# Attention, experts and a dense layer on one core: moving operands prepared over other steps, and a new order of the first slots

## What is computed

```python
# attention, batch 2, 8 heads, 768 tokens, 64 features per head
scores_l = scale * q @ k^T            # kept where |i - j| < 16, else -1e9
scores_s = scale * q @ max(k, blocks of 32)^T + log(32)
a = softmax(concat(scores_l, scores_s))
x = (a @ concat(v, mean(v, blocks of 32)))            # -> x: 1536 tokens x 512
# four experts, hidden 1024 each
x = sum_e p[:, e] * (relu(x @ w1[e]) @ w2[e])         # p: normalised domain_probs
# dense layer, hidden 2048
h = x @ w_in
out = (h * sigmoid(1.702 * h)) @ w_out
```

## Time and profile before

| | us |
|---|---|
| median of 3 runs | 871.56 (871.52 to 872.74) |
| the profiled execution | 872.22 |
| its span in the profile | 870.4 |
| PE busy in the span | 829.6 (95%) |
| POOL busy | 561.2 (64%) |
| DVE busy | 532.2 (61%) |
| ACT busy | 400.1 (46%) |

### The profile page before, as it was taken

The page is one execution under the profiler, slowest core; times in us unless marked ns, Lnnn a source line. Parts: engine busy times, 40 slices in busy tenths (PEclk is TensorE's granted clock), DMA queues, the critical chain, the costliest instruction groups (busy, mean ns, idle before and its releaser), DMA issues.

```text
span 870.4 us, 13892 instructions
## 1 busy us (share of the span) xinstructions
PE 829.6 (95%) x5032; PEld 809.2 (93%) x5032; DVE 532.2 (61%) x1193; ACT 400.1 (46%) x861; POOL 561.2 (64%) x420
## 2 busy tenths in 40 slices
PE   5975999999999999999999999997999998999998
PEld 3765999999999999899999999997999998999998
DVE  4755556666566566566566665664565654566665
ACT  2654544445444444433344333444455545455441
POOL 3567756566556689757556575799466699556550
PEclk9977999999999999999999999999999999999999
DMA  9971242152111211212213121121112121312102
GB/s 270 290 172 55 91 131 83 49 185 78 49 50 55 110 49 57 107 49 99 66 49 116 49 93 53 49 97 49 49 52 94 49 81 66 121 50 97 49 2 73
DMA packets 26420, 74.72 MB, mean 86 GB/s; under 512 B 14704, under 2 KB 15856, under 8 KB 20208
## 3 DMA queue, kind: packets, MB, share of 16 engines
q1 hardware_dynamic: 26352, 73.84, 26.3%
HBM read 70.66 MB, written 3.17 MB: 85 GB/s over the span
## 4 chain that ended last, share of the span: by engine, by line
PE 81%; POOL 9%; issue 4%; ACT 2%; DVE 2%; DMA 1%; SPq 0%; ACTq 0%; DVEq 0%; POOLq 0%
PE bank L1041 26%; PE bank L1043 26%; PE bank L1042 26%; POOL xb_other_lo L527 2%; PE bank L996 1%; POOL t_late L548 1%; DMA k_win<-k_w 1%; POOL wd_lo L513 1%; PE bank L1033 1%; POOL wu_lo L507 1%; PE bank L1007 1%; POOL prob L470 1%; POOL xb_first_lo L527 1%; POOL stage L492 1%; POOL w_sum L490 1%
## 5 line engine op out<-in xcount | busy, mean ns | idle before, releaser
L860 DVE TENSOR_TENSOR xa<-bank,xa 128x384 f32<-128x384 f32 x352 | 195.8, 557 | 219.2 <-PE bank L1043 214.9
L1041 PE MATMUL bank<-h_hi,wd_hi 128*128 128x384 f32 x768 | 258.1, 336 | 0.1
L1043 PE MATMUL bank<-h_lo,wd_hi 128*128 128x384 f32 x768 | 257.7, 335 | 0.0
L1042 PE MATMUL bank<-h_hi,wd_lo 128*128 128x384 f32 x768 | 257.6, 335 | 0.0
L513 POOL TENSOR_TENSOR wd_lo<-stage,wd_hi 128x1024 fp32r<-128x1024 f32 x48 | 115.0, 2396 | 184.9 <-ACT wd_hi L656 184.9
L695 ACT ACTIVATE h_hi<-bank 128x384 fp32r<-128x384 f32 x192 | 94.4, 492 | 224.5 <-DVE bank L891 176.6
L1041 PEld LDWEIGHTS bank<-h_hi,wd_hi 128*128 128x128 f32 x768 | 145.0, 189 | 1.0 <-issue 1.0
L1043 PEld LDWEIGHTS bank<-h_lo,wd_hi 128*128 128x128 f32 x768 | 145.0, 189 | 0.0
L1042 PEld LDWEIGHTS bank<-h_hi,wd_lo 128*128 128x128 f32 x768 | 145.0, 189 | 0.0
L1041 PE MATMUL bank<-xb_other_hi,wu_hi 128*128 128x384 f32 x336 | 112.4, 334 | 5.7 <-ACT snap L679 5.7
L501 POOL TENSOR_TENSOR wu_lo<-stage,wu_hi 128x1024 fp32r<-128x1024 f32 x48 | 114.9, 2395 | 0.0
(11 more groups left out here) (79 smaller groups left out, 1318.4 us busy)
## 6 DMA issues: line engine op xcount, KB each, us to landing
stage<-weights SPq DMA_DIRECT2D x48, 1024.0 KB, 4.9
k_win<-k_w SPq DMA_DIRECT2D x8, 720.0 KB, 8.9
v_win<-v_w SPq DMA_DIRECT2D x8, 576.0 KB, 8.7
q_bd<-q_t SPq DMA_DIRECT2D x16, 192.0 KB, 9.0
p_bc<-p_rows SPq DMA_DIRECT2D x8, 384.0 KB, 4.8
v_cols<-v_t SPq DMA_DIRECT2D x6, 384.0 KB, 6.5
out<-xa SPq DMA_DIRECT2D x4, 384.0 KB, 7.6
out<-xa SPq DMA_DIRECT2D x8, 192.0 KB, 1.9
```

The costliest lines, as they stand in the source:

```text
L860: nc.vector.tensor_tensor(at, y_bank(g, t), at, ALU.add).then_inc(y_taken, 1)
L1041: nc.tensor.matmul(dst, w_h, a_h, start=first, stop=False, skip_group_check=True)
L1042: nc.tensor.matmul(dst, w_l, a_h, start=False, stop=False, skip_group_check=True)
L1043: return nc.tensor.matmul(dst, w_h, a_l, start=False, stop=last, skip_group_check=True)
```

## The change

It does five things. (1) The parts of phases 2 and 3 are made over six steps ahead of the phase (26 to 31, 34 to 39), and nothing of them in the phase's first step; phase 1 keeps its four steps 13 to 16, with its instructions in other places of POOL's and ACT's queues, none of them behind `low_down`. (2) In phase 0 the token halves swap roles (`tokens`), the first step runs its products in the order P1, P5, P6, P2, P7, P4, P3, P1 and P5 of it stand in slots 15 and 16, and the weights of steps 0 and 1 are made earlier in the queues; DVE makes all low parts and sums of phase 0. (3) ACT copies the turned weights of groups 3 to 11, DVE those of 0 to 2. (4) `key_maxima` of a unit stands one slot later, that of unit 1 two slots later; `probs` is loaded ahead of the first values, and `normalize_weights` stands in slot 1. (5) At the end of step 13 ACT runs a sigmoid of one column, before which the sigmoid table is loaded.

```diff
-MADE_0 = (0, 2, 1, 3, 4, 6, 5)
-MADE = (0, 1, 2, 6, 3, 4, 5)
+MADE = (0, 2, 3, 1, 4, 5, 6)
+ORDER_0 = ("P1", "P5", "P6", "P2", "P7", "P4", "P3")
+AHEAD = (None, 3, 6, 6)
...
+        def keys_due(slot):
+            return [1] if slot == GROUPS else [u for u in unit_starting(slot, -1) if u > 1]
...
         def on_act(k):
-            return k >= B_GROUPS or k % 4 == 3
+            return k >= GROUPS
...
+        def tokens(c):
+            return slice(HALF * (1 - c), HALF * (2 - c))
...
         def preparing(g):
-            return next(((ph + 1, g - LAST[ph] + 2) for ph in range(3) if -1 <= LAST[ph] - g < 3), (None, None))
+            return next(((ph, g - FIRST[ph] + AHEAD[ph]) for ph in range(1, 4)
+                         if FIRST[ph] - AHEAD[ph] <= g < FIRST[ph] + (ph == 1)), (None, None))
...
             sp.dma_start(cst[:], consts).then_inc(const_in, 16)
+            sp.dma_start(dp[:], probs.rearrange("(p t) e -> p t e", p=P)).then_inc(dp_in, 16)
...
-            sp.dma_start(dp[:], probs.rearrange("(p t) e -> p t e", p=P)).then_inc(dp_in, 16)
...
 # POOL, slots
-                if slot == 3 + L_X:
+                if slot == 10:
                     sum_weights(0)
-                if slot == 4 + L_X:
+                if slot == 11:
                     low_raw(0)
-                if slot == 5 + L_X:
-                    low_moved(0, 0)
-                if slot == 6 + L_X:
-                    sum_first()
-                if slot == 7 + L_X:
+                if slot == 13:
                     low_sums(0)
-                if slot == 8 + L_X:
-                    low_moved(0, 2)
-            spread_key_maxima(KT)
-            low_down(0)
+                if slot == 14:
+                    low_down(0)
 # POOL, steps
                 ph, part = preparing(g)
-                if part == 3:
-                    low_moved(ph, 4)
+                soon = ph == 1
+                if soon and part == 3:
                     low_moved(ph, 5)
+                    low_moved(ph, 6)
                 if g + 1 < STEPS:
                     sum_weights(g + 1)
+                    if g == 0:
+                        spread_key_maxima(KT)
                     low_raw(g + 1)
...
                 if part == 0:
                     sum_moved(ph, 1)
                 if part == 1:
-                    sum_moved(ph, 2)
+                    low_moved(ph, 2 if soon else 0)
                 if part == 2:
-                    low_moved(ph, 3)
-                    sum_moved(ph, 3)
+                    sum_moved(ph, 4 if soon else 3)
+                if part == 3 and not soon:
+                    sum_moved(ph, 4)
+                if part == 4:
+                    low_moved(ph, 4)
+                if part == 5:
+                    low_moved(ph, 6)
                 if g + 1 < STEPS:
                     low_sums(g + 1)
...
                 if part == 0:
-                    low_moved(ph, 0)
+                    sum_moved(ph, 2)
+                    if soon:
+                        low_moved(ph, 0)
                 if part == 1:
-                    low_moved(ph, 2)
+                    if soon:
+                        sum_moved(ph, 3)
+                        low_moved(ph, 3)
+                    else:
+                        low_moved(ph, 2)
                 if part == 2:
-                    sum_moved(ph, 4)
+                    if soon:
+                        low_moved(ph, 1)
+                        low_moved(ph, 4)
+                    else:
+                        low_moved(ph, 3)
+                if part == 3 and not soon:
+                    low_moved(ph, 1)
+                if part == 4:
+                    low_moved(ph, 5)
                 if g + 1 < STEPS:
                     low_down(g + 1)
-                if part == 0:
-                    low_moved(ph, 1)
-                if part == 1:
-                    low_moved(ph, 6)
...
 # ACT, slots and step 0
-                if slot == 4 + L_X:
+                if slot == 11:
                     high_raw(0)
+                if slot == 12:
+                    high_sums(0)
                     high_moved(0, 0)
-                if slot == 6 + L_X:
-                    high_sums(0)
-                if slot == 7 + L_X:
+                if slot == 14:
+                    high_down(0, 0)
+                    high_down(0, 1)
                     high_moved(0, 2)
-                if slot == 10 + L_X:
-                    high_moved(0, 1)
-            for i in MADE_0[3:]:
+                if slot == 16:
+                    keep(0, 0)
+                    high_moved(0, 3)
+            for i in (1, 4, 5, 6):
                 high_moved(0, i)
-            high_down(0, 0)
-            high_down(0, 1)
+            keep(0, 1)
+            high_raw(1)
+            keep(0, 2)
+            high_hidden(0, "C11")
+            exponent(B_GROUPS)
+            high_sums(1)
...
 # ACT, steps: behind high_sums (first three), behind high_down (last three)
                 if part == 1:
-                    high_moved(ph, 2)
-                if part == 2:
                     high_moved(ph, 3)
+                    if soon:
+                        high_moved(ph, 1)
+                if part == 2 and not soon:
+                    high_moved(ph, 1)
+                if part == 4:
+                    high_moved(ph, 6)
...
                 if part == 0:
-                    high_moved(ph, 1)
-                if part == 1:
+                    high_moved(ph, 2)
+                if part == (1 if soon else 2):
+                    high_moved(ph, 4)
+                if part == (2 if soon else 3):
+                    high_moved(ph, 5)
+                if part == 2 and soon:
                     high_moved(ph, 6)
...
+                if g == ATT_OVER:
+                    act.wait_ge(snap_done, 3 * g + 3)
+                    nc.scalar.activation(sig[:, 0, 0:1], snap[:, 0, 0:1], ACT.Sigmoid).then_inc(table_in, 1)
+                    act.wait_ge(table_in, 1)
...
 # DVE
-                for u in unit_starting(slot, -2):
+                for u in keys_due(slot):
                     key_maxima(u)
...
-                if slot == L_TRANS:
+                if slot == 1:
                     normalize_weights()
-            value_sums(KT)
-            key_maxima(KT)
-            low_moved(1)
+                if slot == 14:
+                    low_moved(0)
+                    sum_first(1)
+                if slot == 15:
+                    low_moved(2)
             sum_first(2)
             sum_first(3)
             low_moved(3)
+            sum_first(4)
+            low_moved(1)
             low_moved(4)
-            sum_first(4)
+            low_moved(5)
             low_moved(6)
-            low_moved(5)
+            key_maxima(KT)
...
+                if g == 0:
+                    mask_scores(B_GROUPS)
+                    value_sums(KT)
...
 # PE
+                if slot == 15:
+                    product(0, "P1")
+                if slot == 16:
+                    product(0, "P5")
+            for name in ("P6", "P2", "P7", "P4"):
+                product(0, name)
+            scores(B_GROUPS)
+            product(0, "P3")
+            turn_value_sums(KT)
+            transpose(B_GROUPS)
```

## The result

The changed kernel takes 851.39 us, median of four runs (850.92 to 852.06), beside 872.15 us for the kernel before on the same chip: a ratio of 0.9757, 95% interval 0.9734 to 0.9779. That is 20.8 us less where 24.6 us less was forecast; the time lies inside the range of 842 to 856 us, 0.4 us above the 851 at which the forecast's own 843 to 851 ends and the second rival's 851 to 856 begins. So the time itself speaks for the second rival as much as for the forecast.

A forecast was written before the change was run, and what follows sets the result against it. PE was taken as gapless except in the attention slots, step 0 and three phase changes, where POOL was late. Gains of 14.4 + 1.9 + 8.3 = 24.6 us gave 847.0 us, forecast band 843 to 851, range 842 to 856.

The forecast's parts named there:

- second rival: Start gives 0 to 4 of 8.3 us, DVE held by POOL or ACT bounding the slots; 851 to 856 us, chance 0.16.
- phases 2 and 3: Phase changes, steps 31 to 36 and 37 to 41: losses of 6.88 and 7.51 us all gone, 14.4 us.
- phase 1: Steps 15 to 17: `sum_weights(17)` comes 1.9 us earlier, 0.3 us of stall left; gain 1.9, bounds 0 and 2.4.
- (a): Slots 1 to 12: shorter DVE queue lets PE run its 2.9 us slots through; gain 2.5 us, bounds 0 and 3.7.
- (b): End of slots, group 11's scores to P1: 14.5 us becomes 12.1, `low_raw(0)` next late; gain 2.4, bounds 0 and 4.
- (c): Step 0, P1 to P1 of step 1: 22.7 us becomes 17.5, limited by a chain through DVE; gain 5.2 us.
- contention: Start: DVE's phase 0 sums and low parts held beside POOL; 1.3 us taken off, bounds nothing and 5.4 us.
- step 1: After step 0: `keep(1, 1)` just late, giving back 0.5 us.
- third rival: Phase changes keep half their loss through a wait between ACT and DVE; 855 to 861 us, chance 0.08.
- Table load: Load moved from step 32 to the end of step 13, where 5.2 us of products cover it; uncovered, 1.3 us once.
- my walk: Step 0 queues: 5.8 us of DVE work after the last group, then group 12 to P1 of step 1; 17.5 us.
- The fourth: Slower: DVE held by POOL without cover in phase 0, 26 us lost; 872 us or above, chance 0.04.

The follow-up runs named there:

- e2_start: The changed kernel with phases 1, 2 and 3 prepared as before, new start and early sigmoid kept: 867.57 us, ratio 0.9948.
- e1_phases: The kernel before with only the new preparation of phases 1, 2 and 3; slots, step 0 and table load as before: 856.69 us, ratio 0.9809.
- e13_late: `e12_down` with POOL's last two parts of phase 1 moved from the head of step 16 to behind `low_raw(17)`: 847.49 us, ratio 0.9715.
- e3_table32: The changed kernel without the one-column sigmoid in step 13, so the table loads in step 32: 851.07 us, ratio 0.9745.
- e5_small: The changed kernel with POOL's `low_down(0)` and `sum_weights(1)` on 8 columns only, leaving out most of their work: 849.3 us, ratio 0.972.
- after_again: The changed kernel run once more, unchanged, as reference for later runs: 851.17 us, ratio 0.9757.
- e12_down: The changed kernel with group 12's scores and mask earlier, and POOL's `low_down(0)` and `low_raw(1)` held until DVE's last low part of phase 0: 848.07 us, ratio 0.972.
- e7_copies: The changed kernel with the turned-weight copies as before, ACT every fourth group and DVE the others: 853.12 us, ratio 0.9766.
- e8_first: The changed kernel with the `probs` load, `normalize_weights` and key maxima back in their old places: 852.66 us, ratio 0.9763.

## Why the prediction was right in kind and 3.8 us off

By its own terms, in the profiled execution of before and of after; the spans differ by 870.4 - 850.3 = 20.1 us:

| term | forecast | measured |
|---|---|---|
| phases 2 and 3 | 14.4 | 14.39 |
| phase 1 | 1.9 | 1.80 |
| (a) slots up to the scores of group 11 | 2.5 | 2.00 |
| (b) these scores to P1 | 2.4 | 1.50 |
| (c) P1 to P1 of step 1 | 5.2 | 1.42 |
| contention | -1.3 | within (b) and (c) |
| step 1 | -0.5 | -0.98 |
| sum | 24.6 | 20.13 |

**Phases.** Right, and by the mechanism named. That the number agrees to 0.1 us is in part how it was made: both sides are read from one profile of before, and the loss of a phase change differs by 1 us or more between executions (`e2_start`). POOL's eleven instructions over six steps, ahead of `low_down`, left no wait behind, and phase 1 kept the two parts at the head of its first step and with them 0.33 us of stall, where 0.3 was forecast. `e1_phases` shows the whole of it with nothing else changed, so the third rival (half of the loss stays) fell. `e13_late` shows that those two parts were the cause of what was left.

**Table load.** The cover was there; the step costs nothing: `keep(12, 2)` at 285.90 to `keep(15, 2)` at 332.70 is 46.80 us, three steps on the beat. The forecast counted the load within phase 2's loss, and `e3_table32` shows that the move was not needed for that: the spreading of POOL's work alone suffices.

**The start: the term that failed is the contention.** I took 1.3 us for DVE beside POOL, "near the lower end, because only the chain after the last group counts, and POOL is then waiting for the keys". Both halves of this reason failed. POOL waits for the keys only while DVE makes the last four low parts, from 63.10 on: up to 62.36 `low_down(0)` and `sum_weights(1)` fill it, and on DVE three low parts and the sums lie beside them. And the chain that counts begins before the last group, because the low part made at 55.43 stands in DVE's queue ahead of everything that follows. Without those POOL instructions P1 to P1 is 17.99 us (`e5_small`); my walk without contention had 17.5. The price was 3.3 us against 21.29, or 2.8 against the 20.76 of `after_again`. The term is mis-sized by 1.5 to 2.0 us in (c) alone. The parts show the same. By the walk the scores of group 12 begin 3.7 + 5.8 + 0.4 = 9.9 us behind P1, and P1 of step 1 another 7.6 us later. In the changed kernel these are 13.08 and 8.21 us, in `e5_small` 10.77 and 7.22. So 3.2 of the 3.8 us that (c) lacks lie ahead of these scores, where DVE works beside POOL. The 17.58 us of `e12_down` are no test of the walk, since that kernel has group 12 in another place. The Trainium skill's rule on the page "GPSIMD Engine Reference", section "Specifications", that POOL contends with DVE instructions that have two SBUF inputs, is borne out: 2.13 us beside POOL, 0.97 without.

(b) lacks 0.9 us. The wait behind `low_raw(0)` was forecast at 1.6 us and is 1.89; PE also waited 1.24 us for ACT's copy of a group's turned weights, which the walk did not have, and `e7_copies` shows that DVE's copies would not have been better. Another part is the contention by the rows, though no run isolates it: PE waited 1.03 us at 53.76 for a normalisation that took 1.70 us instead of the 0.98 of other rows of its kind, beside DVE's low part and sum from 50.43 on.

**(a).** 2.0 instead of 2.5 us; the bounds were 0 and 3.7. How much of that is the change cannot be said to better than 1 to 2 us: in the nine other executions that keep the new start whole, the last scores stand between 42.47 and 43.75, in `e1_phases`, whose start is that of before, at 47.34 against 44.84. Why they differ is not shown. Nor is the mechanism shown that I named for (a), a shorter queue of DVE: `e8_first` puts most of it back and stays within that spread.

**Step 1.** The loss of 0.5 us was forecast for `keep(1, 1)` "just late". No such wait is there: PE has no gap from 76 to 95 us. The 0.98 us are matmuls at half the clock (0.52 us at 77.59, where a matmul at full clock takes 0.34; 1.2 instead of 2.4 GHz), after the idle times of step 0: from P1 to P2 of step 1 pass 3.95 us (77.13 to 81.08), before 2.97 (82.05 to 85.02), and all of the 0.98 lies there. The number was about half of it, the reason was wrong. From P1 of step 1 to `keep(12, 2)` the kernel before takes 207.79 us, the changed kernel 208.77, and `e12_down`, whose P1 of step 1 ran at full clock (0.42), 208.17.

**Rivals.** The second, that the start gives little, came true for the start, in its first mechanism, DVE held by POOL, and at the upper end of its size: 3.9 of the 8.3 us came, where it said 0 to 4, and the time of 851.39 lies in its band. Its other mechanism did not show: ACT did not become the bound of the slots. The fourth, slower than before, had the same mechanism and a price far too high: a DVE instruction of step 0 loses 0.4 to 1.5 us beside POOL, and only those on the chain count. So the forecast was right by the phases, which made 16.2 of the 20.1 us; the start gave less than half of its term, and the range held because it took in the second rival. (The chances that the range leaves out add up to 0.18, where the prediction wrote 0.17.)

**What stays open.** How the 3.2 us of `e12_down` in step 0 divide between its moves, and how each length of step 0 divides between contention and the clock, which differs from one execution to the next (0.74 and 0.83 in two of the changed kernel). And the worth of the new order in the first slots, which lies under what the start varies by from one execution to the next. The new order of the products in step 0 and the exchanged halves of the tokens were never undone alone; they are counted within (b) and (c).

## What to carry to other kernels

When work moves from POOL to DVE to relieve POOL, list what POOL still does in the same microseconds; if both work on two SBUF inputs, let the one that begins later wait for the end of the other, and price that on both engines. Order the queues so that POOL's work that nobody awaits runs after DVE's chain. For work that must be ready at a phase change, first look for the step's own idle time in front of a late producer and put it there, at most as much a step as fits, and none in front of the instruction for which the next engine waits. A beat read from one repeating instruction shows both the loss and what is left of it, to 0.1 us.

## What the runs showed of the hardware that was not expected

DVE and POOL slow each other: the instruction that begins later waits for the other's end and then takes about its usual time, as worked out in the section on the result, and this goes to and fro. Over a stretch the loss falls on both. Beside POOL's `low_down(0)` and `sum_weights(1)` DVE lost 2.9 us (11.49 against 8.55). POOL lost 3.08 + 1.45 + 1.33 + 1.32 + 1.32 = 8.50 against 2.39 + 4 x 0.74 = 5.35, which is 3.15 us. In a single pair it falls on one: `low_sums(0)` at 50.24 lost nothing and the low part at 50.43 lost 1.46 us. So taking work from DVE to POOL or back is priced on both engines, and the prediction had priced only DVE. Its upper bound had the mechanism, DVE held for a POOL instruction each time; it took a value near the lower one. Small instructions suffer as well: in `e5_small` POOL's `low_down(0)` on 8 columns took 0.91 us and ended with DVE's sum, while the sums of 8 columns behind it took 0.20 each:

```profile
56.55 0.91 POOL L527 TENSOR_TENSOR wd_lo<-stage,wd_hi 128x8 fp32r<-128x8 f32 x1
```

DVE's sum there ran from 55.67 to 57.41, and POOL's instruction ended at 57.46. It is the mirror image of the earlier trace rows, where a small DVE instruction ended with POOL's.
